# Six of eight weight tiles transposed on VectorE in 32x32 blocks instead of on TensorE, and the last output tile by halves

## What is computed

```
q_bucket, k_bucket = sign bits of q @ proj, k @ proj, as numbers
attn = softmax(where(q_bucket == k_bucket, q @ k.T / 8, -1e9)) @ v       # per head
x    = attn, heads side by side                                           # 1536 x 512
y    = ((x @ w1) * (x @ w2)) @ w3 @ w_out          # w1, w2 512x1024, w3 1024x1024, w_out 1024x512
out  = sum over e of p[:, e] * (relu(y @ moe2_w1[e]) @ moe2_w2[e])        # 4 experts
```

## Time and profile before

| | us |
|---|---|
| median of 3 runs (lowest, highest) | 982.63 (982.26, 983.13) |
| the profiled execution | 981.78 |
| its span | 980.0 |
| around the span | 1.78 |

### The profile page before, as it was taken

One profiled execution on the slowest core, in us unless ns is written; L12 is line 12 of the kernel. 1 busy time (PEld: TensorE's weight loads), 2 busy tenths in 40 slices (PEclk: granted clock), 3 DMA queues, 4 the chain that ended last, 5 costly groups with the idle time before them and its releaser, 6 DMA issues.

```text
span 980.0 us, 15717 instructions
## 1 busy us (share of the span) xinstructions
PE 973.1 (99%) x5385; PEld 904.4 (92%) x5385; DVE 591.2 (60%) x955; ACT 455.3 (46%) x844; POOL 355.9 (36%) x348
## 2 busy tenths in 40 slices
PE   8999999999999999999999999999999999999998
PEld 6889999999999999999998988989889899898997
DVE  4469999999987780678654453443624435354442
ACT  4258888888885552555540331413404134042230
POOL 1113564556764320335171340512505226043130
PEclk9999999999999999999999999999999999999999
DMA  8436877765445330301110201102010020100102
GB/s 256 125 76 159 213 210 200 207 169 135 109 146 159 113 113 1 112 2 44 44 44 1 65 22 43 43 1 66 22 43 27 16 63 22 43 22 21 43 28 101
DMA packets 89869, 81.55 MB, mean 83 GB/s; under 512 B 33376, under 2 KB 72416, under 8 KB 89824
## 3 DMA queue, kind: packets, MB, share of 16 engines
q1 hardware_dynamic: 89824, 80.97, 29.5%
HBM read 54.69 MB, written 7.39 MB: 63 GB/s over the span
## 4 chain that ended last, share of the span: by engine, by line
PE 98%; DVE 1%; DMA 1%; SPq 0%; issue 0%; ACT 0%
PE ps L315 25%; PE ps L316 25%; PE ps L317 25%; PE ps L1521 6%; PE ps L1508 4%; PE ps L1536 3%; PE ps L1538 3%; PE ps L1510 3%; PE ps L1487 1%; PE ps L1469 1%; PE ps L1418 1%; PE ps L1475 1%; PE ps L1478 1%; DMA stage<-in_moe_w_out 1%; DVE expo L1089 0%; DVE pT_lo L1103 0%
## 5 line engine op out<-in xcount | busy, mean ns | idle before, releaser
L702 POOL TENSOR_TENSOR v_sum<-kept,kept 128x384 f32<-128x384 f32 x48 | 49.1, 1022 | 355.3 <-ACT kept L857 355.3
L857 ACT COPY kept<-ps 128x384 f32<-128x384 f32 x144 | 68.5, 478 | 213.8 <-PE ps L317 212.9
L1383 DVE SCALAR_TENSOR_TENSOR acc<-ps,gate,acc 128x512 f32<-128x512 f32 x96 | 72.0, 750 | 140.1 <-PE ps L317 140.1
L317 PE MATMUL ps<-v_hi,hid_lo 128*128 128x512 f32 x384 | 149.6, 390 | 0.0
L316 PE MATMUL ps<-v_lo,hid_hi 128*128 128x512 f32 x384 | 149.5, 389 | 0.0
L315 PE MATMUL ps<-v_hi,hid_hi 128*128 128x512 f32 x384 | 149.4, 389 | 0.0
L1232 DVE TENSOR_TENSOR u_sum<-ps,kept 128x384 f32<-128x384 f32 x48 | 26.8, 557 | 122.7 <-PE ps L317 122.7
L1089 DVE TENSOR_SCALAR_CACHE_REDUCE expo<-ps 128x768 f32<-128x768 f32 x96 | 91.7, 956 | 14.1 <-PE ps L1510 10.6
L788 ACT ACTIVATE expo<-expo,neg_max 128x768 f32<-128x768 f32 x96 | 90.5, 942 | 8.0 <-DVE expo L1089 5.8
L1103 DVE TENSOR_TENSOR pT_lo<-ps,pT_hi 128x768 fp32r<-128x768 f32 x96 | 90.5, 947 | 3.7 <-ACT pT_hi L802 3.4
L802 ACT CAST pT_hi<-ps 128x768 fp32r<-128x768 f32 x96 | 76.6, 798 | 24.8 <-PE ps L1521 24.5
(11 more groups left out here) (164 smaller groups left out, 2368.5 us busy)
## 6 DMA issues: line engine op xcount, KB each, us to landing
w_raw<-gate_sums SPq DMA_DIRECT2D x16, 512.0 KB, 3.6
e_raw<-in_moe_w SPq DMA_DIRECT2D x64, 128.0 KB, 2.3
v_raw<-in_moe_w SPq DMA_DIRECT2D x32, 256.0 KB, 3.3
w_raw<-in_moe_w SPq DMA_DIRECT2D x48, 128.0 KB, 3.5
made_raw<-in_moe_w SPq DMA_DIRECT2D x16, 256.0 KB, 3.6
gate_sums<-made SPq DMA_DIRECT2D x8, 512.0 KB, 2.7
raw_qk<-in_q SPq DMA_DIRECT2D x16, 192.0 KB, 3.0
raw_qk<-in_k SPq DMA_DIRECT2D x16, 192.0 KB, 3.4
```

Of the source, the lines that this page charges most:

```text
L317: return nc.tensor.matmul(out_ps, lhs_lo, rhs_hi, start=False, stop=stop, skip_group_check=onto)
L702: nc.gpsimd.tensor_tensor(v_sum[:, :], kept[s][1][:, :], kept[s][2][:, :], ALU.add).then_inc(v_done, 1)
L857: nc.scalar.copy(kept[s][n][:, :], ps[4 * s + n][:, 0:HALF]).then_inc(kept_done, 1)
L1383: nc.vector.scalar_tensor_tensor(acc[:, t, :], ps[4 * ((h + t // 4) % 2) + t % 4], gate_f[:, bass.ds(t * E + e, 1)], acc[:, t, :], ALU.mul ...
```

## The change

1. PE transposes only w3's tiles 0 and 1. Tiles 2 to 7 are transposed by DVE, one `nc.vector.transpose` per tile (`turn_w3`), which turns each 32x32 block of the tile in place of its position; hence the blocks must already lie in transposed positions when they land.
2. So each of tiles 2 to 7 is loaded by eight transfers (4 groups of 32 partitions x 2 halves, each 32 rows x 4 blocks x 128 columns, 64 KB in pieces of 512 bytes) in place of one. Their waits: tiles 2 and 3 as before on PE's transposes of tiles 0 and 1; tiles 4 to 7 on DVE's `w3_turned`.
3. In SP's order, tile 2's load now stands ahead of the q and k of head 0, tile 3's just behind them, and both ahead of the constants. The wait of tile 2's load therefore stands where q's and k's issue was.
4. In DVE's order, `turn_w3(2)` and `turn_w3(3)` stand ahead of `w3T_low(2)`, and `turn_w3(it + 2)` at the end of each pass, which in the pass with it = 2 is ahead of `constants()`. ACT and DVE split these tiles from SBUF, not from PSUM.
5. DVE's turning leaves the rows of w3's transpose in another order within each half (row 4p + k at partition p of block k). w_out's blocks are loaded in the same order (rows 8 KB apart, 2 KB each, still 256 KB a transfer), and PE's transposes of tiles 0 and 1 read their columns with a stride of four elements.
6. The last output tile is made in two halves of 256 columns: 24 matmuls of 256 columns in place of 12 of 512, the second half into another bank; two adds on DVE, two stores of 128 KB. To this end PE's last expert is taken out of its loop.

```diff
@@ SP
-                sp.dma_start(stage[kt][:, :], moe_w_out[kt * P:(kt + 1) * P, :]).then_inc(stage_loaded[kt], 16)
+                sp.dma_start(stage[kt][:, :], wout_tiles[kt // 4, kt % 4, :, :]).then_inc(stage_loaded[kt], 16)
...
             def load_w3(it, par):
-                sp.wait_ge(w3T_mm, w3T_count(it - 2, 2) if isinstance(it, int) else 2 * (it - 1))
-                sp.dma_start(w3_raw[par][:, :], w3_tiles[it, :, :]).then_inc(w3_loaded[par], 16)
-
+                if it < 2 + PE_TILES:
+                    sp.wait_ge(w3T_mm, w3T_count(it - 2, 2))
+                else:
+                    sp.wait_ge(w3_turned, it - 1 - PE_TILES)
+                for a in range(BLOCKS):
+                    raw = w3_raw[par][a * BLOCK:(a + 1) * BLOCK, :].rearrange("i (b h c) -> i b h c", b=BLOCKS, h=2)
+                    for h in range(2):
+                        sp.dma_start(raw[:, :, h, :], w3_blocks[it, a, :, :, h, :]).then_inc(w3_loaded[par], 16)
+
+            load_w3(2, 0)
             load_qk(0, 0, True)
+            load_w3(3, 1)
             sp.dma_start(proj_f[0:DH, :], proj).then_inc(const_loaded, 16)
...
-            load_w3(2, 0)
-            load_w3(3, 1)
             load_v(0, 0, True)
             load_qk(0, 1, True)
             load_v(0, 1, True)
-            with sp.Fori(2, FK // 2) as m:
-                for par in range(2):
-                    load_w3(2 * m + par, par)
+            for it in range(4, FK):
+                load_w3(it, it % 2)
@@ ACT, w3T_high
+                if it < PE_TILES:
...
+                else:
+                    act.wait_ge(w3_turned, it + 1 - PE_TILES)
                     act.wait_ge(wp_mm, it - 1)
@@ DVE
+            def turn_w3(it, par):
+
+                dve.wait_ge(w3_loaded[par], 16 * 2 * BLOCKS * (it // 2))
+                if it >= 2 + PE_TILES:
+                    dve.wait_ge(w3T_lo_done, w3T_count(it - 2, 2))
+                nc.vector.transpose(w3T_raw[par][:, :, :].rearrange("p (h k) (b i) -> p b h k i", h=2, i=BLOCK),
+                                    w3_raw[par][:, :].rearrange("p (b h j k) -> p b h k j", b=BLOCKS, h=2, j=BLOCK))\
+                    .then_inc(w3_turned, 1)
...
+            turn_w3(2, 0)
+            turn_w3(3, 1)
             for half in halves(2):
                 w3T_low(2, 0, half)
...
                 if it < FK - 1:
                     w3T_low(it + 1, (it + 1) % 2)
+                if it + 2 < FK:
+                    turn_w3(it + 2, it % 2)
                 if it == 2:
                     constants()
@@ PE
             multiply_wp(0, 0, (6, 7))
-            for half in halves(2):
-                transpose_w3(2, 0, False, half)
             multiply_wp(1, 1, (6,))
...
                 if it < FK - 1:
-                    transpose_w3(it + 1, (it + 1) % 2, False)
                     first_prep(2 * it - 1)
...
+                        for n, cols in enumerate(tile_parts(last and h == ROUNDS - 1, t)):
+                            if n:
+                                pe.wait_ge(acc_done, ALL_TILES * r + 8)
```

More of the change, by code:

```diff
@@ L111, in build_program @@
         wout_lo = place("wout_lo", [P, FK * D], F32R, wout_at)
+        w3T_raw = [place(f"w3T_raw{n}", [P, FK, P], F32, wout_at) for n in range(2)]
         assert s_raw_at[0] <= cursor[0] and wout_at[0] <= cursor[0]
@@ L311, in up_unit, with tile_parts, down_bank @@
             return GATE_UNITS + ROUND_STEPS * (ROUNDS * e + h) + j
+        def tile_parts(last, t):
+            return (slice(0, D // 2), slice(D // 2, D)) if last and t == ALL_TILES - 1 else (slice(0, D),)
+        def down_bank(h, t, n):
+            t -= 4 * n
+            return ps[4 * ((h + t // 4) % 2) + t % 4]
         def mult3(out_ps, lhs_hi, lhs_lo, rhs_hi, rhs_lo, start, stop, onto=False):
@@ L862, in _ @@
             first, second = halves(0)
-            w3T_high(0, 0, True, first)
+            w3T_high(0, 0, first)
             wout_high(0)
-            w3T_high(1, 1, True, first)
+            w3T_high(1, 1, first)
             for j in range(1, 5):
                 wout_high(j)
-            w3T_high(0, 0, True, second)
+            w3T_high(0, 0, second)
             wout_high(5)
-            w3T_high(1, 1, True, second)
+            w3T_high(1, 1, second)
             wout_high(6)
@@ L879, in _ @@
             for half in halves(2):
-                w3T_high(2, 0, False, half)
+                w3T_high(2, 0, half)
             wp_high(0)
@@ L1058, in w3T_low @@
                 dve.wait_ge(w3T_hi_done, w3T_count(it, hi))
-                nc.vector.tensor_tensor(part(w3T_lo[par]), ps_w3T[par][:, lo:hi, :], part(w3T_hi[par]).bitcast(F32),
+                src = ps_w3T[par][:, lo:hi, :] if it < PE_TILES else part(w3T_raw[par])
+                nc.vector.tensor_tensor(part(w3T_lo[par]), src, part(w3T_hi[par]).bitcast(F32),
                                         ALU.subtract).then_inc(w3T_lo_done, hi - lo)
+            def turn_w3(it, par):
[5 more added lines that the diff above has]
+                    .then_inc(w3_turned, 1)
             def wp_low(it):
@@ L1641, in _ @@
             pe.wait_ge(ident_ready, 1)
-            transpose_w3(0, 0, True, first)
+            transpose_w3(0, first)
             run_on_zeros(2)
-            transpose_w3(1, 1, True, first)
+            transpose_w3(1, first)
             begin_wp(0, 0)
@@ L1722, in multiply_y, with expert @@
                         part(n, ft, ft == 0, ft == FT_ORDER[-1])
-            def expert(e, first):
+            def expert(e, first, last):
                 for h in range(ROUNDS):
@@ L1751, in expert @@
                             pe.wait_ge(acc_done, ALL_TILES * r + t - 7)
[L1752 to L1758 removed]
+                        for n, cols in enumerate(tile_parts(last and h == ROUNDS - 1, t)):
+                            if n:
+                                pe.wait_ge(acc_done, ALL_TILES * r + 8)
+                            for p in range(PIECES):
+                                if t == 0:
+                                    pe.wait_ge(v2_lo_done, PIECES * r + p + 1)
+                                done = mult3(down_bank(h, t, n)[:, cols], hid_hi[:, B * p + b, toks],
+                                             hid_lo[:, B * p + b, toks], v2_hi[p][:, cols], v2_lo[p][:, cols],
+                                             p == 0, p == PIECES - 1)
+                            done.then_inc(down_mm, 1)
             for b in range(B):
@@ L1762, in _ @@
                 multiply_y(b)
-            expert(0, True)
-            with pe.Fori(1, E) as e:
-                expert(e, False)
+            expert(0, True, False)
+            with pe.Fori(1, E - 1) as e:
+                expert(e, False, False)
+            expert(E - 1, False, True)
 def bucket_codes(bits):
```

58 lines of the change are left out of this document (28 added, 30 removed).

## The result

| | before | after |
|---|---|---|
| median (lowest, highest), us | 981.98 (981.48, 983.13), 6 runs | 991.12 (990.19, 993.38), 6 runs |
| profiled execution / its span | 981.78 / 980.0 | 990.19 / 988.2 |

The ratio is 1.0094, with a 95% interval of 1.0081 to 1.0107. The forecast was 991.6, the range 986.0 to 996.0. The profiled execution is the fastest of the six.

A forecast was written before the change was run, and what follows sets the result against it. PE, 99% busy, was taken as the bound, with SP's queue deciding the change. Profiled 981.78 + 9.3 (tile 7 late) - 0.3 (end) = 990.8; the median lies 0.85 above, so 991.6 us, range 986.0 to 996.0.

The forecast's parts named there:

- An issue: SP's queue: each new w3 transfer takes 0.58 us to issue, bounds 0.46 and 0.68; eight a tile, 24 on the path.
- Landing: Time until a w3 tile's transfers have landed: 2.8 us, bounds 2.3 and 3.7.
- The constants: SP's queue: six constants at 0.56 us each; up to 1.6 us extra for the first as an upper bound.
- SP's restart: SP stands still from 6.83 until tile 0's second-half transposes end at 12.29 us, then issues tile 2's load.
- The turn: DVE's transposition of a w3 tile takes 1.25 us, between 1.1 and 2.4, doubling because reads jump by four elements.
- The clock: Rival, chance 0.15: PE's idle stretches lower the clock, slowing tile 3's matmuls by 2.7 to 5.45 us; 994.3 us.
- Given back: PE's saved transposes return 0.8 us ahead of tile 4, 0.1 ahead of tile 5, 0.8 ahead of tile 6.
- Row order: w_out's other row order taken as 0; the strided read in 16 PE transposes 0 to 1.6 us, taken as 0.
- Splits from SBUF in place of PSUM: ACT's and DVE's splits of the turned tiles cost 0: same elements, beside matmuls, with room on both engines.
- The end: Last output tile by halves: shorter add, PE's 256-column matmuls and smaller store give -0.3 us, from -0.5 to +1.4.
- The rival of cheap issues: Rival, chance 0.12: SP issues at the bare 0.33 us, 24 issues take 6.0 us less; 985.6 us.
- Faster after all: Rival, chance 0.07: SP's issues cost so little that loads hide and only PE's saving counts, 3.6 us; 979.0 us.

The follow-up runs named there:

- e5: Changed kernel with DVE's turn reading contiguous columns instead of every fourth one: 992.01 us in one run, a turn 1241 ns against 1999.
- e7: Kernel before with only w_out's rows in the new order and PE's strided transposes: 983.46 us, ratio 1.0012.
- e6: Changed kernel with own buffers for w3's tiles 2 to 5, SP's and DVE's orders altered, tile 0's result split earlier: 985.32 us, ratio 1.0027.
- e9: e6 with the load of v of head 0 moved to just behind q and k: 982.70 us, ratio 1.0007.
- e10: e9 with six small matmuls on zeros in place of two ahead of tile 1's first transposes: 982.51 us, ratio 1.0006.
- e12: e10 with `turn_w3(3)` ahead of `constants()` on DVE: 981.90 us, ratio 1.0006.
- e1: Changed kernel with q, k and the constants issued on SP ahead of w3's tiles 2 and 3 again: 988.65 us, ratio 1.0070.
- e2: Changed kernel with `constants()` ahead of `turn_w3(4)` on DVE: 989.23 us, ratio 1.0068.
- e8: Changed kernel with the order changes of e1 and e2 together: 989.45 us, ratio 1.0066.

## Why the prediction was right, and where its terms were not

The sign, the place and the size held: SP's queue stood still from 6.7 to 12.7 us, PE idled ahead of tile 2 and ahead of `first_prep(4)` for the buffers named, and tile 7 and everything behind it was shifted, by 8.6 us where 9.3 were forecast. Term by term:

- **An issue:** 0.58 taken, 0.46 to 0.50 measured, the low bound. Twenty-four of them are some 2.4 us less. **Landing:** 2.8 taken, 2.1 measured (23.32 for tile 3, whose last issue began about 21.2); it counts once, for tile 4. **The constants:** the first took 0.52 us, and the extra of up to 1.6 did not come. (10.54 to 13.25 in the earlier trace rows is 0.54 for each of five, not 0.56; that is 0.1 us over the six.) **SP's restart:** 12.29 taken, 12.67 measured.
- **The turn:** 1.25 taken, 2.0 measured. The doubling named as the upper bound was nearer; e5 shows that the contiguous price, 1.24, was right and that the stride adds 0.76. The prediction's estimate of 1.07 us, from the Trainium skill, Vector Engine (DVE) Microarchitecture Reference, section 3.8, lies under even the contiguous turn.
- Together (-2.4, -0.7, +0.7, +0.4, and some -0.2 in `constants()`) these put tile 3's matmuls at 38.6, where 40.8 had been forecast: 8.9 late, not 11.0. The stalls were 4.6 and 1.4 us, where 6 and 4.8 had been forecast; the second is 2.3 us shorter for tile 2's matmuls, which ran slow into it (7.8 us in place of 5.45).
- **The clock** was the rival with 0.15, at +2.7 on the forecast (994.3 against 991.6). It happened, twice. The first fall was hidden, as the rival said, since tile 2's matmuls end ahead of the next stall; the second made tile 3's take 7.2 us and not 5.6: 1.5, less than the rival's lower bound, since 8 of the 24 were slow and not half. This step failed: the forecast left the clock out of its sum, calling the trace silent, although the Trainium skill's rule (TensorE: Matmul & The Clock Gate, Why this matters for your kernels) stood beside it. That the number is so near is in part luck: 1.5 us of clock stood against 2.2 us by which the path to tile 3 had been taken too long.
- **Given back:** 0.8 ahead of tile 4 (there, under the clock's +1.5: 8.9 to 9.5 late), 0.1 ahead of tile 5 (0.0), 0.8 ahead of tile 6 (0.85).
- **Row order:** 0 taken, 1.2 measured by itself (e7). The bound of 1.6 covered it, but it named PE's strided reads; a group of four of these now takes 0.39 us up to the next matmul in place of 0.35. What the traces show late is the landing of w3's second tile. From 3 to 5 us the DMA engines were as busy as before (0.85 and 0.83) for little more than half the bytes; in e7 they moved still less (108 GB/s at 0.56). So the unpriced term was most likely w_out's new pieces; e7 changed both at once, and the two were not tried apart. On the path of the profiled execution the term shows only as the 0.4 us of SP's restart.
- **Splits from SBUF in place of PSUM:** 0 taken. On DVE and ACT that held, and the changed kernel has no wait from it; but it is not free beside POOL (last section).
- **The end:** -0.3 taken, -0.45 in the trace; 256 columns took 0.12 us a matmul, as taken, and no weight load set the pace.

The range of the main case was not added up alike on both sides: its lower terms together give 988.3, as stated, its upper ones 997.7 and not 995.5. Nothing measured lay there.

The rival of cheap issues (0.33 us, 985.6) is out; no eight w3 issues in a row took under 0.456 each. Faster after all is out as a forecast for this kernel, and the versions whose loads come early (e6, e9, e10, e12) did not reach 979 either. Their traces suggest why, though no run takes the parts one from another: the 3.3 us that the forecast counted for the transposes stand against the row order (1.2) and waits of 2.2 to 3.4 us around `first_prep(4)` and tile 3, whose cause changed from run to run: POOL in e6, the bits in e9 and e10, `proj_lo` and the bits in e12.

Not settled: how much of the change's 9.1 us each order bears when the other is there, since e1, e2 and e8 came out within 1 us of each other; what DVE's order around `turn_w3(3)` alone would give back of the 4.6 us ahead of tile 2, since `first_prep(4)` would then wait the longer for `proj_lo`; and why the first matmuls of some executions run at half rate up to 13 us (0.43 us apart in the traces of e2 and e9, while the granted clock reads 1.00 there).

## What to carry to other kernels

Before moving work from the engine that bounds a kernel, count the issues that its new layout needs on the one queue that feeds everything, and where in that queue the first waiting one stands: 48 issues of 0.47 us in place of six, behind a standstill of 6.0 us and with DVE's and SP's orders as they were, made the kernel 9.1 us slower, where a group of eight transposes saved 0.8. The same 48 issues without the standstill and with other orders left 3.1 us (e6) and then, with v in time, 1.1 (e9): it was less their number than what stood behind them. In an engine's program, too, put nothing that waits for a late transfer ahead of work that another engine is waiting for, as `turn_w3(3)` stood ahead of tile 2's low parts. In an early stage with no slack, a repair moves the stall to the next engine in program order, so look at what is queued in front of the late operand (v in front of q_main, the turn in front of the constants) before counting on the gain. Price a strided read by a run of its own, and an idle stretch of the matmul engine together with the slow matmuls behind it.

## What the runs showed of the hardware that was not expected

- DVE and POOL hold each other up. Four `proj_lo` of 64x6 elements took 0.74 us in the kernel before and 2.92 and 3.01 us in e9 and e10, where they fell beside POOL's q_main and q_cross; the longest single one took 1.80 us, where q_cross takes 1.85. In the kernel before, q_cross ended at 25.11 and `proj_lo` began at 25.96. In e12, where the same four ran at 28.75, behind q_cross, they took 0.74 again. It works the other way too: q_cross of head 1, beside a w3T_lo, took 1.84 us in the kernel before, where w3T_lo reads PSUM, and 2.82 in the changed kernel, where it reads SBUF. The Trainium skill, SBUF — State Buffer, SBUF: two separate sides, says that a VectorE operation with two SBUF inputs and a GpSimd operation that reads SBUF lock each other out for a whole instruction; these rows agree.
- A DVE transpose of 128x1024 words takes 1.24 us on contiguous reads and 2.0 us where it reads every fourth element.
- A wait of PE of 2.2 us (e10, ahead of tile 3) went with a granted clock of 0.79 in 28 to 36 us, and tile 3's matmuls took 7.1 us; e12's profile, with 1.7 and 1.0 us in two waits there, kept 1.00, and they took 5.6 us. In the changed kernel waits of 1.4 and 0.7 us came ahead of the second fall.
